# Thirty products of zeros on TensorE ahead of the first attention scores

## The reference

```python
def reference(**kwargs):
    ...
    attn_out = _attn_ref(**attn_kwargs)      # q, k, v: (2, 8, 768, 64)
    B, H, S, D = attn_out.shape
    x = np.ascontiguousarray(attn_out.transpose(0, 2, 1, 3)).reshape(B * S, H * D)
    x = _moe_ref(x=x, **moe_kwargs)          # (silu(x @ w_gate) * (x @ w_val)) @ w_out, width 1536
    return _moe2_ref(x=x, **moe2_kwargs)     # h = x @ w_in, piecewise square, @ w_out, width 2048
```

## Time and profile before

| what | value |
|---|---|
| time, median of 3 runs | 614.23 us (613.68 to 614.72) |
| the profiled execution's own time | 614.17 us |
| its span, first to last instruction | 612.4 us |
| TensorE busy, matmuls | 588.3 us, 96% of the span |
| VectorE busy | 469.8 us, 77% |
| ScalarE busy | 365.1 us, 60% |
| GpSimd busy | 87.2 us, 14% |
| data moved by DMA | 59.77 MB |

### The profile page before, as it was taken

How to read it: one execution, slowest core, us unless ns; L and a number is a source line. 1 busy time by engine, 2 the same in 40 slices (tenths; PEclk the granted TensorE clock), 3 DMA queues, 4 the chain that set the end, 5 groups by cost and what they waited for, 6 DMA issues and landing times.

```text
span 612.4 us, 10207 instructions
## 1 busy us (share of the span) xinstructions
PE 588.3 (96%) x3720; PEld 539.3 (88%) x3720; DVE 469.8 (77%) x914; ACT 365.1 (60%) x735; POOL 87.2 (14%) x78
## 2 busy tenths in 40 slices
PE   2889999999999999999999999999999999999997
PEld 2466789999899999999999999998878899998886
DVE  6578698888866757888766757997998479979843
ACT  4883888988755445556645445665565356665522
POOL 4452134333310002222210000000000000000000
PEclk9989999999999999999999999999999999999999
DMA  9998235334112202223212202321211323011212
GB/s 330 290 284 265 84 109 146 106 113 147 36 52 69 70 1 71 81 88 123 86 36 70 70 1 68 130 87 59 69 52 52 138 70 118 4 36 69 70 52 103
DMA packets 32961, 59.77 MB, mean 98 GB/s; under 512 B 3280, under 2 KB 7376, under 8 KB 32912
## 3 DMA queue, kind: packets, MB, share of 16 engines
q1 hardware_dynamic: 32384, 58.21, 29.9%
q10 hardware_dynamic: 528, 0.92, 0.6%
HBM read 54.53 MB, written 3.15 MB: 94 GB/s over the span
## 4 chain that ended last, share of the span: by engine, by line
PE 80%; DVE 9%; SPq 3%; DMA 3%; issue 2%; ACT 2%; POOL 0%; ACTq 0%; POOLq 0%; DVEq 0%
PE ps L526 45%; PE ps L663 17%; PE ps L635 15%; DMA k_raw_b<-k_t_dram 3%; DVE hid_lo L1165 1%; SPq L380 1%; PE ps L516 1%; PE ps L487 1%; DVE rel L1171 1%; DVE x_lo L1097 1%; DVE h L1174 1%; SPq L359 1%; PE ps L494 1%; DVE t_first L1089 1%; DVE t_late L1089 1%
## 5 line engine op out<-in xcount | busy, mean ns | idle before, releaser
L526 PE MATMUL ps<-x_hi,w_hi 128*128 128x384 f32 x560 | 191.2, 341 | 2.6 <-ACT part L862 1.4
L526 PE MATMUL ps<-x_lo,w_hi 128*128 128x384 f32 x560 | 187.4, 335 | 0.0
L526 PE MATMUL ps<-x_hi,w_lo 128*128 128x384 f32 x560 | 187.3, 334 | 0.0
L526 PEld LDWEIGHTS ps<-x_hi,w_hi 128*128 128x128 f32 x560 | 105.1, 188 | 6.8 <-issue 5.0
L526 PEld LDWEIGHTS ps<-x_hi,w_lo 128*128 128x128 f32 x560 | 105.2, 188 | 0.4 <-issue 0.2
L526 PEld LDWEIGHTS ps<-x_lo,w_hi 128*128 128x128 f32 x560 | 105.1, 188 | 0.0
L896 ACT ACTIVATE wout_hi<-wout_raw 128x512 fp32r<-128x512 f32 x56 | 35.3, 631 | 95.1 <-PE ps L663 52.0
L663 PE MATMUL ps<-wout_hi,hid_hi 128*128 128x512 f32 x192 | 74.8, 390 | 0.8 <-DVE wout_lo L1159 0.8
L663 PE MATMUL ps<-wout_hi,hid_lo 128*128 128x512 f32 x192 | 75.2, 392 | 0.1
L663 PE MATMUL ps<-wout_lo,hid_hi 128*128 128x512 f32 x192 | 74.8, 390 | 0.0
L1159 DVE TENSOR_TENSOR wout_lo<-wout_raw,wout_hi 128x512 fp32r<-128x512 f32 x56 | 39.4, 704 | 40.1 <-ACT wout_hi L896 39.6
(11 more groups left out here) (105 smaller groups left out, 917.6 us busy)
## 6 DMA issues: line engine op xcount, KB each, us to landing
w_raw<-w_dram SPq DMA_DIRECT2D x80, 256.0 KB, 2.9
wout_raw<-w_dram SPq DMA_DIRECT2D x56, 256.0 KB, 2.6
out_dram<-y_out SPq DMA_DIRECT2D x12, 256.0 KB, 2.1
k_a<-k_t_dram SPq DMA_DIRECT2D x6, 384.0 KB, 7.0
v_s<-v_rows_dram SPq DMA_DIRECT2D x6, 384.0 KB, 15.0
v_a<-v_rows_dram SPq DMA_DIRECT2D x6, 384.0 KB, 4.5
k_raw<-k_t_dram SPq DMA_DIRECT2D x3, 512.0 KB, 4.6
q_a<-q_t_dram SPq DMA_DIRECT2D x6, 256.0 KB, 6.8
```

Source lines behind the costliest of these rows:

```text
L526: last = nc.tensor.matmul(dst, lhs, rhs, start=start and kk == 0 and i == 0, stop=kk == 1 and i == 2, skip_group_check=not start)
```

## The change

TensorE gets 30 products at the head of its list, before the scores of tile 0. Each multiplies a 128x128 block of `masked` by itself, 128 columns, into the first 128 columns of the bank `v_sum_ps[0]`; nothing reads the result. VectorE gets one memset, ahead of all its others, which fills that block with zeros and releases TensorE through a new semaphore.

```diff
+WARM = 30
...
+        zeros_ready = sem("zeros_ready")
...
+            pe.wait_ge(zeros_ready, 1)
+            for i in range(WARM):
+                nc.tensor.matmul(v_sum_ps[0][:, 0:P], masked[:, 0, 0], masked[:, 0, 0], start=True, stop=True)
 
 
             for s in range(LAST_A):
...
+            nc.vector.memset(masked[:, 0, 0], 0.0).then_inc(zeros_ready, 1)
             nc.vector.memset(ident[:], 0.0)
             nc.vector.memset(mask[:, :, 0:WIN], 0.0)
             nc.vector.memset(sel[:], 0.0).then_inc(filled, 1)
```

## The result

The changed kernel takes 615.70 us in the median of 19 runs (614.74 to 617.17), the kernel before 613.98 in its 19 (613.30 to 615.51). The ratio is 1.0030, with a 95% interval of 1.0022 to 1.0037: slower by 1.8 us by the ratio, where no change was forecast. The profiled execution took 617.10 with a span of 615.2; 2.9 us more than the one of before. It is among the slowest of the 19, so a second profile was taken of the same kernel (after_again: 615.93, span 614.1).

What follows compares the result with a forecast made beforehand. The prediction took k_raw_b's transfer, landing at 41.08 us, as the early bound, then VectorE's fixed order, then TensorE's long stages. Tiles within 0.48 us of spare time cost nothing: 614.17 + 0 = 614.2 us, range 613.2 to 616.5.

Steps and rivals of the forecast that it cites:

- The products ended: Head of TensorE's list: the 30 products of zeros were to end at 10.8 us, bounds 9.1 to 11.4.
- the first mask: Tile 0's mask after its scores: to come at 11.5 us in place of 10.28, 1.3 late.
- the tiles stood: Batch 0's attention tiles behind 23 us: 1.3 late less 1.4 given back, -0.1 us, bounds -1.8 to +0.5.
- The pace at 2.4 GHz: Products of zeros at the high clock: one record each 0.13 us taken, lower bound 0.11; at the low clock 0.22.
- the clock rose later: During TensorE's products: the rise was taken at 5.6 us, halfway between cases of 3.9 and 7.3.
- the reading of VectorE's list: VectorE from 41.10 to 59.90: busy 18.54 of 18.80 us in fixed order, with TensorE's long stages behind.
- What reaches the end: Tiles against k_raw_b's landing at 41.10: only lateness beyond 0.48 us counts, 0 in the middle, 0.02 at the upper bound.
- what is queued hides a later issue: SyncE's transfers ahead of k_raw_b's landing: with 18.66 us queued, an issue one microsecond later finds the engines still at work.
- The part-by-part account: Costs of memset, products, moved tiles, time given back and what reaches the end; they summed to 0 us.
- the clock that falls again: Rival: in TensorE's gap before the transposes at 16.0 the clock drops, 1.4 to 3.1 us lost, 615.6 to 617.3; chance 0.20.
- Zeros do count: Answers a rival: products of zeros don't wake TensorE's clock, 2.0 to 4.8 us reach the end, 616.2 to 619.0; chance 0.05.
- the tiles were not the bound: Answers a rival: tiles, not the landing, bound the kernel, so 1.8 us go through to the end, 612.4; chance 0.06.

Runs made afterwards that it cites:

- memset_only: The changed kernel without its products (WARM = 0), keeping the memset, the semaphore and TensorE's wait; 613.85 us, ratio 0.9990 to 1.0009.
- tiny30: The changed kernel with its 30 products cut to 32 output rows and 4 columns: the same 120 instructions, nearly no work; 616.01 us, ratio 1.0021 to 1.0045.
- tiny12: tiny30 with 12 products in place of 30, so 48 added instructions; 614.00 us, ratio 0.9985 to 1.0006.
- wide7: The changed kernel with 7 products of 512 columns (28 instructions) in place of 30 of 128, memset widened to 512 columns; 616.02 us, ratio 1.0013 to 1.0041.
- wide7_fill: wide7 plus three 512-column filler products behind TensorE's wait for the probabilities, ahead of tile 11's transposes; 618.71 us.
- wide7_order: wide7 with VectorE's list reordered: copies out of tiles 5 to 7 and others before the first reduction of k_raw_b; 614.91 us, ratio 1.0006 to 1.0025.
- before_order: The kernel before with the same new VectorE order as wide7_order and no products of zeros; 616.16 us, ratio 1.0019 to 1.0044.
- tiny30_b: The same kernel as tiny30, profiled once more; 616.0 us in one run.
- wide5: wide7 with 5 products of 512 columns in place of 7, so 20 added instructions; 613.98 us, ratio 0.9992 to 1.0010.
- wide7_fill2: wide7 plus three 512-column filler products ahead of TensorE's wait for tile 11's transposes; 615.57 us, ratio 1.0013 to 1.0032.

## Why the prediction was wrong

Its numbers for TensorE and the tiles held. The products ended at 10.68 (10.8 taken), the first mask was at 11.46 (11.5), the tiles stood 0.37 us early at 22 (0.1 taken, within the bounds). The memset was free (memset_only). The pace at 2.4 GHz was the lower bound: the changed kernel's L674 in two windows has 14 records in 3 us and then 20 in 2, with the one in progress at either end, so about 0.21 and 0.11 us (0.22 and 0.13 were taken). The column of the clock reads 1.00 in both, as it did in the kernel before.

```profile
1.05:4.05 3.00, 3.00 (x14) 3.00 (x15) 1.00 0.71 212
7.40:9.40 2.00, 2.00 (x20) 2.00 (x19) 1.00 1.07 400
```

That the end came so near 10.8 is partly luck, for two misses cancel. The fast records are quicker than taken, and the clock rose later: 25 records start in the 5.35 us from 1.05, so it rose near 6.6 and not at 5.6. after_again shows how much this moves: there it rose near 5.1, after 18 records, and the products ended at 9.98.

And the time behind the landing is as fixed as the reading of VectorE's list said: 571.3 us in the kernel before, 571.2 to 571.4 wherever VectorE's order was kept and the clock did not fall between 41 us and the end.

The step that failed is the one under "What reaches the end": "Nor is anything gained by being early, since the landing doesn't move", and with it the argument that what is queued hides a later issue. The issue moved from 22.42 to 23.60, the flight stayed at 18.7 us, and the landing moved by 1.2 us; through VectorE's fixed order all of it reached the end, and the clock's fall added up to 1.6 us. The prediction had named this sign itself: a landing more than 0.5 us from 41.1. The part-by-part account left out what instructions are besides work: 120 of them are 120 to be fetched, and the transfers of instructions (q8) share the 16 engines that were the bound. I had read the transfers for the order of their issue and not for who else uses the engines; the page's list of queues has 30 transfers of 16 KB of instructions, with 0.3% of the engines' time. That 120 instructions alone bring the fetch forward, the issue of `k_raw_b` back by 1 us and the time up by 1.3 to 2.8 us is shown (tiny30 against tiny12 and memset_only). How the fetch holds up the transfers is argued from `v_tok_a` and SyncE's rows.

The second gap is the early tiles' own effect. wide7 has no early fetch, issues `k_raw_b` at 22.51 as the kernel before does, and still starts the reduction at 41.76 and is 1.7 us slower. Its profiled execution divides into 0.7 us of landing and 0.7 of the clock's fall after 3.05 us in which TensorE is idle. The landing's part is weak evidence. The kernels with early tiles and no early fetch land at 41.49 to 41.74 (wide7, wide7_fill, wide7_order), those without either at 40.29 to 41.09; but before_order, whose tiles are late, landed at 41.51. So that early tiles delay the landing is not shown, nor how they might: the transfers that ScalarE issues start 0.4 us earlier, at 25.0, and may compete with SyncE's, but no run here changed that alone. The clock's fall is not theirs alone either: in tiny30_b and after_again, with late tiles, the late landing left 1.81 and 2.37 us of idle time before the same transposes, and the clock fell. Nor do the two effects add: the changed kernel has both and is not slower than either.

Of the rivals, the clock that falls again was seen (after_again, at 15 to 19 us) and wide5 shows it too; it isn't what cost the time, though after_again's 615.93 lies in the rival's range: VectorE still waited for the landing there, and wide5 is as quick as the kernel before. Zeros do count as work for the clock (the records of zeros went from 0.21 to 0.11 us apart), and the tiles were not the bound (VectorE waited 2.04 and 3.12 us).

The Trainium skill, "Runtime: NRT & Kernel Launch", "Instruction fetch mechanics", says that each engine's instructions are refilled in blocks of 16 KiB, 256 instructions, by a DMA queue of its own, and calls the cost mostly hidden. The size agrees with the q8 rows. The cost does not: it is hidden from TensorE, whose value sums take their usual 1.88 us while the changed kernel's fetch is under way at 16.3, and falls on the transfers in the full queues, 0.8 to 1.5 us for the last of `v_tok_a`.

The Trainium skill, "TensorE: Matmul & The Clock Gate", "HAM oscillation — how this bites in real kernels", describes a wait for DMA long enough to throttle TensorE, with the next burst starting slow. The changed kernel's trace agrees in its place (3.60 us idle, then 1.2 GHz to 51), though this gap was made by the change that was to bring the clock up early.

## What to carry to other kernels

Instructions added in a stretch that DMA bounds are not free because their engine is idle: enough of them (120 here, not 48) bring the next fetch of instructions forward, a transfer of about 1.1 us, and transfers in flight behind it land as much later. Few long instructions leave the fetch where it was (wide5, wide7), though wide7 gained nothing by it. Look at which queue carries instructions before costing an edit at nothing. And ask first what a gain would run into: work that ends earlier ahead of a fixed landing only makes the gap longer, and on TensorE a gap can cost the clock (0.5 to 1.6 us here).

## What the runs showed that was not expected

- One fetch of 16 KB, 1.1 us long, goes with a whole transfer of 512 KB that lands 1.1 us late: the first two of `v_tok_a` unchanged, the third from 10.5 to 11.6 us.
- wide7_fill2 differs from wide7 only behind 41 us, and yet its first 16 KB fetch lies ahead of 22 us and that of wide7 behind it. So where a fetch falls is not a matter of the instructions ahead of it alone; why was not settled.
- 48 added instructions cost nothing (614.00), 120 cost 1.3 to 2.8 us (616.01), 256 cost 0.1 to 1.7 (615.77). Twice as many cost no more: it looks like a step where the fetch moves, not a slope.
- The sum of span less the landing's first use is 571.2 to 571.4 us in all ten profiles (of eight kernels) that keep VectorE's order and have no fall of the clock between 41 us and the end, and is a sharper measure than the time.
